# Identity products between the attention matmuls of the first slots, and the first loads issued from two engines

## The chip, the cores and the metric

One core of one Trainium2 chip runs the whole program in one launch. The metric is the device time of one execution in microseconds (us); lower is better. The core has TensorE (PE, the matrix engine), VectorE (DVE), ScalarE (ACT), GpSimd (POOL) and SyncE (SP), each with its own instruction stream, coupled by semaphores; 16 DMA engines move data between HBM and the on-chip memory. The kernel uses DMAs that SP, ACT or POOL start.

## The reference, cut to what matters

Three stages follow one another for each of 4 batches, all in fp32:

```python
# attention: 8 heads, 768 positions, head size 48
for t in range(S):
    state = alpha[:, :, t, :, None] * state + einsum('bhd,bhe->bhde', k[:, :, t], v[:, :, t])
    y[:, :, t] = einsum('bhd,bhde->bhe', q[:, :, t], state)
# token and channel mixer on x = y as (4, 768, 384)
u = x + (relu(xT @ w_tok1) @ w_tok2)T          # 768 -> 256 -> 768
x = u + relu(u @ w_ch1) @ w_ch2                # 384 -> 1536 -> 384
# channel mix with a shift by one position
k = relu(xk @ w_k); out = sigmoid(xr @ w_r) * ((k * k) @ w_v)
```

## The kernel before

**Attention in slots.** A batch's attention is cut into 6 chunks of 128 positions (c) times 4 pairs of heads (p), 24 steps in all; step i is chunk i // 4, pair i % 4. A pass over one batch has 28 slots. In each slot every engine does its share of several steps at once: in the first pass (r = 0) slot s holds the transposes of step s, the scores of step s - 2 and the output of step s - 3 (`steps_of`). Each engine's order is written out by hand in its `attention_part`. On TensorE, in slot s of the first pass:

- `attention_scores` (L519, L523): one transpose of the decayed keys and one fp32 product of 96 rows by 256 columns, after ScalarE has written `qbd`.
- `transposes` (L505): three fp32 transposes of q, k and alpha of a pair of heads, each by the identity `ident`. The first step waits for `consts_g` >= 3 (the identity is made by GpSimd), `consts_v` >= 2 and `pair_loaded` >= 48, the next one and then every fourth for `qka_loaded` of its chunk.
- `attention_out` (L543, L547, L550): four products of 48 columns, from chunk 1 on one of 96 columns with the running state, and one of 96 columns for the state.

VectorE does, per slot: the mask (L931, after the scores), the two scans of alpha (L896, L898, after the transposes), L905, L908 and L911 that scale q and k, then the state (L942 or L945) and the low part of the output (L950). ScalarE spreads q (L757, after L911), copies keys (L751) and the high part of the output (L747). GpSimd masks the state (L418) and makes the low parts of the weights (L412).

**The first pass stands alone.** In r = 0 nothing but attention runs, beside the loading and splitting of the mixer's weights, and, after slots 10, 14, 18 and 22 and at the end, three or six products of 384 columns, `early_token_up` (L588). In passes 1 to 3 each slot of attention is interleaved with a slot of the mixer of the batch before (L577, L608, L620, L636), which is much more matmul work. After pass 3 comes the mixer of the last batch, then the channel mix.

**Loads.** All loads of the first pass are issued by SP, in program order, and the waits in between are SP's own: first q, k and alpha of the first two heads of chunk 0 (L320, `pair_loaded`), then q, k, alpha of its other six heads (L300, `qka_loaded[0]`) and its v (L308), two pieces of weights (L317), then chunk 1, two more pieces, chunk 2, and mu (L328). Later chunks are loaded every fourth slot. Three buffers hold chunks 0, 1 and 2 (`chunk_buffer`). ScalarE issues no DMA. TensorE's results go to eight banks; `b_ring[1]` is a bank that nothing uses in the first pass before the mixer begins.

Of the kernel before, what the change touches and what calls it, by code (L numbers as in the profile page):

```python
# [13 lines left out]
def attention_mixer_channel_mix(nc, q, k, v, alpha, w_tok1, w_tok2, w_ch1, w_ch2,  # L14
# [7 lines left out]
    P = 128  # L22
    B, H, S, D = q.shape
# [28 lines left out]
    with ctx:  # L52
        def sb(name, shape, dt=F32):
            return ctx.enter_context(nc.sbuf_tensor(name, shape, dt))
# [29 lines left out]
        def wr_w(n, kt):  # L84
# [26 lines left out]
        ident = sb("ident", [P, P])  # L111
# [8 lines left out]
        qka3 = [[words[:, n * DM:(n + 1) * DM].rearrange("p (h d) -> p h d", h=H) for n in range(3)]  # L120
                for words in (qka[0], qka[1], free_words[0])]
        qbd = free_words[1][:, 0:4 * P].rearrange("p (n t) -> p n t", n=2)
        vt3 = [vt[0][:, :], vt[1][:, :], mixed[:, 0, :]]
# [9 lines left out]
        b_ring = [bank[3], bank[4]]  # L133
# [32 lines left out]
        consts_g = sem("consts_g")  # L166
# [3 lines left out]
        pair_loaded = sem("pair_loaded")  # L170
        qka_loaded = [sem(f"qka_loaded{n}") for n in range(3)]
        v_loaded = [sem(f"v_loaded{n}") for n in range(3)]
# [99 lines left out]
        def is_first(r):  # L272
            return isinstance(r, int) and r == 0
# [7 lines left out]
        @block.sync  # L281
        def _(sp):
            def last_use(r, c):

                if is_first(r):
                    return NP * (c - 2)
                if c >= 2:
                    return STEPS * r + NP * (c - 1)
                if isinstance(r, int) and r == 1:
                    return NP * (NC - 2 + c)  # L290
                return STEPS * (r - 1) + NP * (NC - 1 + c)

            def load_qka(b, r, c):

                buf, _ = chunk_buffer(r, c)
                if not is_first(r) or c >= 3:
                    sp.wait_ge(tr_done, last_use(r, c))
                for n, t in enumerate((q, k, alpha)):
                    h0 = 2 if is_first(r) and c == 0 else 0
                    sp.dma_start(qka3[buf][n][:, h0:H, 0:D],  # L300
                                 t[b, h0:H, c * P:(c + 1) * P, :].rearrange("h p d -> p h d"))\
                      .then_inc(qka_loaded[buf], 16)

            def load_v(b, r, c):
                buf, _ = chunk_buffer(r, c)
                if not is_first(r) or c >= 3:
                    sp.wait_ge(y_done, last_use(r, c))
                sp.dma_start(vt3[buf].rearrange("p (h d) -> p h d", h=H),  # L308
                             v[b, :, c * P:(c + 1) * P, :].rearrange("h p d -> p h d")).then_inc(v_loaded[buf], 16)

            def load_piece(n):
                dst, loaded, _ = staging(n)
                if n >= NALL - 2:
                    sp.wait_ge(tile_done, TILES * (B - 1) + KT + 2 * KC)
                elif n >= NRAW:
                    sp.wait_ge(w_lo_ready, n - NRAW + 1)
                sp.dma_start(dst.rearrange("p (k n) -> p k n", k=piece_size(n)[0]), PIECES[n][0]).then_inc(loaded, 16)  # L317

            for n, t in enumerate((q, k, alpha)):
                sp.dma_start(qka3[0][n][:, 0:2, 0:D], t[0, 0:2, 0:P, :].rearrange("h p d -> p h d"))\  # L320
                  .then_inc(pair_loaded, 16)
            for c in range(3):
                load_qka(0, 0, c)
                load_v(0, 0, c)
                for n in range(NRAW * c // 2, min(NRAW * (c + 1) // 2, NRAW)):
                    load_piece(n)
            for n, m in enumerate((mu_k, mu_r)):
                sp.dma_start(mu[:, n, :], m.rearrange("(c p) -> p c", p=P),  # L328
                             allow_slow_non_contiguous=True).then_inc(mu_loaded, 16)

            for s in range(SLOTS):

                rc, c = divmod(s // NP + 2, NC)
                if s % NP == 0 and s > 0 and (rc, c) < (1, 1):
                    load_qka(rc, rc, c)
                rc, c = divmod((s - 3) // NP + 2, NC)
                if (s - 3) % NP == 0 and s > 3 and (rc, c) < (1, 1):
                    load_v(rc, rc, c)
                for n in pieces_in(s):
                    if n + NRAW < NMIX:  # L340
                        load_piece(n + NRAW)
            load_qka(1, 1, 1)
            load_v(1, 1, 1)

            def load_chunks(r, first, last):
                for c in range(first, last):
                    load_qka(r, r, c)
                    load_v(r, r, c)

            with sp.Fori(1, B - 1) as r:  # L350
                load_chunks(r, 2, NC)
                load_chunks(r + 1, 0, 2)
            load_chunks(B - 1, 2, NC)


            for n in range(NMIX, NALL):
                load_piece(n)


            def load_x2(b, half):  # L360
                sp.wait_ge(x2_stored[half], 16 * b + 16)
                lo = half * HT - half
                sp.dma_start(x2_in[half][:, :, 1 - half:HT + 1],
                             x2_dram[b, :, lo:(half + 1) * HT].rearrange("(c p) t -> p c t", p=P))\
                  .then_inc(x2_loaded[half], 16)

            def store_out(b, half):
                for m in range(TM):
                    sp.wait_ge(y_ready, TM * (2 * b + half) + m + 4)
                    t0 = half * HT + m * P  # L370
                    sp.dma_start(out[b, t0:t0 + P, :], y_out[:, m, :]).then_inc(y_stored[m], 16)
                for m in range(TM):
                    sp.wait_ge(y_stored[m], 16 * (2 * b + half + 1))
                sp.sem_inc(y_free, 1)

            sp.wait_ge(consts_v, 6)
            for half in range(2):
                load_x2(0, half)
            with sp.Fori(0, B - 1) as b:
                for half in range(2):  # L380

                    sp.wait_ge(mixed_ready, 2 * KC * (2 * b + half + 1))
                    load_x2(b + 1, half)
                    store_out(b, half)
            for half in range(2):
                store_out(B - 1, half)
# [100 lines left out]
        @block.tensor  # L487
        def _(pe):
            PASSES = ((0, 0), (0, 1), (1, 0))

            def transposes(r, i):
                c, p = step(i)
# [16 lines left out]
            def attention_scores(r, i):  # L509
# [14 lines left out]
                else:  # L524
                    pe.wait_ge(split_ready, 3 * (STEPS * (r - 1) + i + 1))
                    for n, (a, b) in enumerate(PASSES):
                        mm = nc.tensor.matmul(scores, ks[a][0:W2, :], qs[b][0:W2, :], start=(n == 0), stop=(n == 2))  # L527
# [27 lines left out]
            def attention_part(r, s):  # L555
                tr, sc, yo = steps_of(r, s)
                if not is_first(r) and yo is not None:
                    attention_out(r, yo)
                if sc is not None:
                    attention_scores(r, sc)  # L560
                if tr is not None:
                    transposes(r, tr)
                if is_first(r) and yo is not None:
                    attention_out(r, yo)
# [6 lines left out]
            def token_up(b, m):  # L571
# [3 lines left out]
                for n in range(3 * NC):  # L575
                    i, j = PASSES[n // NC]
                    mm = nc.tensor.matmul(dst, tok1_w(i, n % NC, m), x[j][:, n % NC, :],  # L577
# [3 lines left out]
            def early_token_up(c):  # L581
# [4 lines left out]
                pe.wait_ge(xlo_ready, NP * (c + 1))  # L586
                for k, (i, j) in enumerate(PASSES):
                    mm = nc.tensor.matmul(b_ring[0][:, 0:HT], tok1_w(i, c, 0), x[j][:, c, :],  # L588
# [4 lines left out]
            def token_down(b, half, m):  # L593
# [7 lines left out]
                for n in range(3 * KT):  # L601
                    kt, (i, j) = n // 3, PASSES[n % 3]
                    if t == KT:
# [8 lines left out]
            def channel_up(b, j):  # L612
# [5 lines left out]
                for n in range(3 * KC):  # L618
                    a, c = PASSES[n // KC]
                    mm = nc.tensor.matmul(dst, ch1_w(a, n % KC, jj), u[c][:, n % KC, half * HT:(half + 1) * HT],  # L620
# [20 lines left out]
            def mixer_part(b, s):  # L641
# [7 lines left out]
                else:  # L649
# [3 lines left out]
                    if s > FIRST_UNIT:  # L653
                        channel_down(b, s - FIRST_UNIT - 1)

            for s in range(SLOTS):
                attention_part(0, s)
                if s >= 2 * NP + 2 and (s - 2) % NP == 0:
                    early_token_up((s - 2) // NP - 2)
            early_token_up(NC - 1)  # L660
# [62 lines left out]
        def _(act):  # L723
# [88 lines left out]
            def mix_next(nxt, half):  # L812

                if nxt is not None:
                    for n in range(KC + 1):
                        mix_step(nxt, half, n, 0, KC - 1)

            for s in range(SLOTS):
                attention_part(0, s)
                for n in pieces_in(s):  # L820
                    split_hi(n)
# [302 lines left out]
```

## Time and profile before

| what | us |
|---|---|
| median of 3 runs | 779.77 |
| lowest, highest | 778.67, 794.02 |
| the profiled execution, its own time | 785.57 |
| its span from the first to the last instruction | 783.9 |
| TensorE busy | 768.6 (98%) |
| VectorE, ScalarE, GpSimd busy | 469.9, 303.3, 127.7 |

The profiler recorded one execution. The page gives the busy time of each engine, the span in 40 equal slices with the granted clock of TensorE (PEclk, tenths of full speed; full is 2.4 GHz), the DMA queues, and the chain that ended last, followed back from the last instruction. Besides the page, the trace can be asked for instructions in order of time, for the chain of waits in order of time, for busy time by stretch, and for who waited for whom. Ends of matmuls are modelled since they are pipelined, so a busy TensorE is not one at its peak; the distance from start to start is the safer measure.

### The profile page before, as it was taken

What the parts mean: (1) busy time and instruction counts of PE and PEld (TensorE: products, weight loads), DVE (VectorE), ACT (ScalarE), POOL (GpSimd) and SP (SyncE); (2) the same over time, 40 slices, a digit from 0 to 9 for tenths busy, and PEclk for the clock granted to TensorE, in tenths of its full rate; (3) what the DMA queues carried; (4) which work ended last, traced back from release to release, by engine and by line L of the source; (5) the groups of instructions that cost most, each with busy time, mean ns of one, the idle gap of its engine ahead of it and who ended that gap; (6) DMA issues with size and microseconds to landing.
All of it is one profiled execution on the core that took longest, in us unless ns stands there. A gap on an engine that the chain in (4) does not pass through costs nothing.

```text
span 783.9 us, 13623 instructions
## 1 busy us (share of the span) xinstructions
PE 768.6 (98%) x4792; PEld 755.0 (96%) x4792; DVE 469.9 (60%) x1379; ACT 303.3 (39%) x843; POOL 127.7 (16%) x174
## 2 busy tenths in 40 slices
PE   6999999999999999999999999999899999999998
PEld 5988899999999999999999999999899999999998
DVE  5696877773777776387777431334663653653751
ACT  3475333332333333143333222234653643643641
POOL 1475333110013210012311043001000000000000
PEclk9999999999999999999999999999999999999999
DMA  9675222222122222122240004201010110110000
GB/s 201 142 176 127 42 41 43 71 41 41 41 56 46 42 71 42 40 43 41 41 108 18 1 31 152 73 5 61 11 50 31 41 50 30 40 50 30 5 26 30
DMA packets 114502, 43.77 MB, mean 56 GB/s; under 512 B 101776, under 2 KB 111632, under 8 KB 114448
## 3 DMA queue, kind: packets, MB, share of 16 engines
q1 hardware_dynamic: 113296, 38.36, 20.4%
q0 software_dynamic: 1152, 4.72, 1.6%
q8 instruction: 31, 0.51, 0.3%
q14 instruction: 23, 0.19, 0.1%
HBM read 33.63 MB, written 9.44 MB: 55 GB/s over the span
## 4 chain that ended last, share of the span: by engine, by line
PE 87%; DVE 8%; ACT 3%; issue 1%; DMA 0%; SPq 0%; DVEq 0%; ACTq 0%
PE bank L636 19%; PE bank L620 18%; PE bank L701 13%; PE bank L679 12%; PE bank L688 4%; PE bank L543 4%; PE bank L505 4%; PE bank L527 3%; PE bank L547 2%; PE bank L577 2%; PE bank L523 2%; PE bank L550 2%; PE bank L608 2%; ACT qs_hi L757 1%; DVE qs_lo L921 1%
## 5 line engine op out<-in xcount | busy, mean ns | idle before, releaser
L757 ACT ACTIVATE qs_hi<-qkd,rhead 96x128 fp32r<-96x128 f32 x144 | 50.1, 395 | 152.2 <-DVE qkd L911 152.2
L975 DVE SCALAR_TENSOR_TENSOR hid_lo<-bank,hid_hi 128x384 fp32r<-128x384 f32 x96 | 52.8, 550 | 68.2 <-ACT hid_hi L765 68.2
L418 POOL TENSOR_TENSOR state<-state,own 96x96 f32<-96x96 f32 x80 | 31.0, 388 | 258.7 <-DVE state L945 183.2
L765 ACT ACTIVATE hid_hi<-bank 128x384 fp32r<-128x384 f32 x96 | 46.0, 479 | 68.9 <-PE bank L620 68.9
L620 PE MATMUL bank<-u_hi,wch_hi 128*128 128x384 f32 x288 | 71.4, 356 | 0.0
L851 ACT ACTIVATE relu_k<-bank 128x384 f32<-128x384 f32 x64 | 31.5, 491 | 101.2 <-PE bank L679 83.5
L921 DVE SCALAR_TENSOR_TENSOR qs_lo<-qkd,rhead,qs_hi 96x128 fp32r<-96x128 f32 x144 | 45.9, 358 | 35.5 <-ACT qs_hi L757 35.5
L620 PE MATMUL bank<-u_lo,wch_hi 128*128 128x384 f32 x288 | 65.8, 336 | 0.0
L636 PE MATMUL bank<-hid_lo,wch_hi 128*128 128x384 f32 x288 | 65.5, 335 | 0.0
L620 PE MATMUL bank<-u_hi,wch_lo 128*128 128x384 f32 x288 | 65.5, 335 | 0.0
L636 PE MATMUL bank<-hid_hi,wch_hi 128*128 128x384 f32 x288 | 65.4, 334 | 0.0
L636 PE MATMUL bank<-hid_hi,wch_lo 128*128 128x384 f32 x288 | 65.4, 334 | 0.0
L1091 DVE TENSOR_TENSOR x_half<-bank,x_half 128x384 f32<-128x384 f32 x24 | 13.4, 557 | 76.0 <-PE bank L701 74.7
L543 PEld LDWEIGHTS bank<-vt,relu_k 128*128 128x128 f32 x352 | 54.0, 203 | 1.9 <-DVE relu_k L931 1.8
L747 ACT ACTIVATE x_hi<-bank 128x96 fp32r<-128x96 f32 x96 | 23.8, 248 | 79.5 <-PE bank L550 62.5
L1074 DVE TENSOR_TENSOR relu_k<-relu_k 128x384 f32<-128x384 f32 x64 | 35.7, 558 | 27.8 <-ACT relu_k L851 24.8
L505 PE MATMUL bank<-ident,qka 128*96 128x128 f32 x264 | 46.4, 287 | 5.8 <-DMA qka<-in_alpha 5.8
L543 PE MATMUL bank<-vt,relu_k 128*128 128x48 f32 x352 | 50.9, 270 | 0.8 <-DVE relu_k L931 0.8
L620 PEld LDWEIGHTS bank<-u_lo,wch_hi 128*128 128x128 f32 x288 | 51.7, 188 | 0.0
L620 PEld LDWEIGHTS bank<-u_hi,wch_lo 128*128 128x128 f32 x288 | 51.5, 188 | 0.0
L636 PEld LDWEIGHTS bank<-hid_hi,wch_hi 128*128 128x128 f32 x288 | 51.2, 188 | 0.1
L636 PEld LDWEIGHTS bank<-hid_hi,wch_lo 128*128 128x128 f32 x288 | 51.3, 188 | 0.0
(116 smaller groups left out, 1799.0 us busy)
## 6 DMA issues: line engine op xcount, KB each, us to landing
w_raw<-in_moe_w_ch SPq DMA_DIRECT2D x12, 384.0 KB, 3.3
x_scratch<-x_half POOLq DMA_DIRECT2D x8, 576.0 KB, 3.5
out<-x_half SPq DMA_DIRECT2D x24, 192.0 KB, 1.9
vt<-in_v SPq DMA_DIRECT2D x22, 192.0 KB, 2.7
qka<-in_q SPq DMA_DIRECT2D x21, 192.0 KB, 2.8
qka<-in_k SPq DMA_DIRECT2D x21, 192.0 KB, 3.6
qka<-in_alpha SPq DMA_DIRECT2D x21, 192.0 KB, 3.8
qka<-x_scratch SPq DMA_DIRECT2D x4, 577.5 KB, 3.9
```

What stands on the lines that cost most here:

```text
L505: mm = nc.tensor.transpose(transposed_qka(r, i)[:, n * P:(n + 1) * P], qka3[qb][n][:, 2 * p:2 * p + 2, :].rearrange("p h d -> p (h d)"), i ...
L543: mm = nc.tensor.matmul(y_ps[:, h * D:(h + 1) * D], am[:, i % 2, h * P:(h + 1) * P], vt3[vb][:, p * W2 + h * D:p * W2 + (h + 1) * D], star ...
L620: mm = nc.tensor.matmul(dst, ch1_w(a, n % KC, jj), u[c][:, n % KC, half * HT:(half + 1) * HT], start=(n == 0), stop=(n == 3 * KC - 1))
L636: mm = nc.tensor.matmul(b_acc[m][:, 0:HT], ch2_w(a, jj, m), hid[c][:, j % HJ, :], start=(jj == 0 and n == 0), stop=(jj == NJ - 1 and n == 2))
L679: mm = nc.tensor.matmul(dst, wk_w(a, n % KC, j), mix_out[0][c][:, n % KC, :], start=(n == 0), stop=(n == 3 * KC - 1))
L701: mm = nc.tensor.matmul(bank[m][:, 0:DM], k2[a][:, n % NF, m * P:(m + 1) * P], wv_w(c, n % NF), start=(n == 0), stop=(n == 3 * NF - 1))
L757: nc.scalar.activation(dst[0:W2, h * P:(h + 1) * P], qkd[0:W2, first_of(i), :], ACT.Copy, scale=rhead[0:W2, i % 4, h:h + 1])\
L765: nc.scalar.activation(dst, b_ring[t % 2][:, 0:HT], func).then_inc(tile_hi, 1)
L851: nc.scalar.activation(relu_k[:, j % 2, :], b_ring[j % 2][:, 0:HT], ACT.Relu)\
L921: nc.vector.scalar_tensor_tensor(qs[1][0:W2, cols], qkd[0:W2, first_of(i), :], rhead[0:W2, i % 4, h:h + 1], qs[0][0:W2, cols], ALU.mult, A ...
L975: ins = nc.vector.scalar_tensor_tensor(dst, src, 0.0, hi, ALU.max, ALU.subtract)
L1074: nc.vector.tensor_tensor(relu_k[:, j % 2, :], relu_k[:, j % 2, :], relu_k[:, j % 2, :], ALU.mult).then_inc(k2_ready, 1)
```

## The change

ScalarE's stream now begins with three DMA issues: k of the first two heads of chunk 0, k of its other six heads, and v of chunk 0. SP issues q and alpha of the first two heads, then q and alpha of the other six, then goes straight to the first pieces of weights and to chunk 1. TensorE waits at its start for the identity, and issues four products of the identity by itself (fp32, 128 by 128, into `b_ring[1]`, which nobody reads), two more after slot 0, and one after each of slots 1 to 5: eleven in all. No engine waits for them otherwise.

```diff
-                    h0 = 2 if is_first(r) and c == 0 else 0
-                    sp.dma_start(qka3[buf][n][:, h0:H, 0:D],
-                                 t[b, h0:H, c * P:(c + 1) * P, :].rearrange("h p d -> p h d"))\
+                    sp.dma_start(qka3[buf][n][:, :, 0:D], t[b, :, c * P:(c + 1) * P, :].rearrange("h p d -> p h d"))\
                       .then_inc(qka_loaded[buf], 16)
...
-            for n, t in enumerate((q, k, alpha)):
+            for n, t in ((0, q), (2, alpha)):
                 sp.dma_start(qka3[0][n][:, 0:2, 0:D], t[0, 0:2, 0:P, :].rearrange("h p d -> p h d"))\
                   .then_inc(pair_loaded, 16)
+            for n, t in ((0, q), (2, alpha)):
+                sp.dma_start(qka3[0][n][:, 2:H, 0:D], t[0, 2:H, 0:P, :].rearrange("h p d -> p h d"))\
+                  .then_inc(qka_loaded[0], 16)
             for c in range(3):
-                load_qka(0, 0, c)
-                load_v(0, 0, c)
+                if c > 0:
+                    load_qka(0, 0, c)
+                    load_v(0, 0, c)
...
+            WARM = (4, 2, 1, 1, 1, 1, 1)
...
+            def keep_warm(count):
+
+                for _ in range(count):
+                    nc.tensor.matmul(b_ring[1][:, 0:P], ident[:, :], ident[:, :], start=True, stop=True)
+
+            pe.wait_ge(consts_g, 3)
+            keep_warm(WARM[0])
             for s in range(SLOTS):
                 attention_part(0, s)
+                if s + 1 < len(WARM):
+                    keep_warm(WARM[s + 1])
...
+            act.dma_start(qka3[0][1][:, 0:2, 0:D], k[0, 0:2, 0:P, :].rearrange("h p d -> p h d"))\
+               .then_inc(pair_loaded, 16)
+            act.dma_start(qka3[0][1][:, 2:H, 0:D], k[0, 2:H, 0:P, :].rearrange("h p d -> p h d"))\
+               .then_inc(qka_loaded[0], 16)
+            act.dma_start(vt3[0].rearrange("p (h d) -> p h d", h=H),
+                          v[0, :, 0:P, :].rearrange("h p d -> p h d")).then_inc(v_loaded[0], 16)
             for s in range(SLOTS):
                 attention_part(0, s)
```

## Rows read from the trace of the kernel before

**Rows 1.** The page: head, busy time, granted clock in 40 slices
```profile
span 783.9 us, 13623 instructions
...
PE 768.6 (98%) x4792; PEld 755.0 (96%) x4792; DVE 469.9 (60%) x1379; ACT 303.3 (39%) x843; POOL 127.7 (16%) x174
...
PEclk9999999999999999999999999999999999999999
```

**Rows 2.** Busy time by stretch: span, us busy per engine (instructions), PEclk, DMA share, GB/s
```profile
13.70:33.00 19.30, 19.30 (x85) 17.28 (x85) 13.69 (x50) 9.26 (x28) 7.17 (x11) 1.00 0.83 186
40.00:60.00 20.00, 19.54 (x150) 17.52 (x149) 19.64 (x81) 14.04 (x46) 16.15 (x18) 1.00 0.72 178
```

**Rows 3.** Chain of waits in order of time, slots 4 to 12: start us, us, what
```profile
13.74 0.73 PE bank L505 x3
...
25.57 0.64 PE bank L505 x3
...
28.82 0.64 PE bank L505 x3
...
38.64 0.33 PE bank L505 x3
```

**Rows 4.** The same chain, slot 14 and VectorE's mask of two slots, four apart
```profile
42.01 0.34 PE bank L505 x3
...
48.88 0.36 DVE relu_k L931
...
56.88 0.36 DVE relu_k L931
```

**Rows 5.** Instructions of TensorE in order of time, products of L588: start us, us
```profile
34.44 0.52 PE L588 MATMUL bank<-x_lo,wtok_hi 128*128 128x384 f32 x1
```

**Rows 6.** All engines in order of time, slot 26 and after
```profile
59.21 0.33 PE L588 MATMUL bank<-x_lo,wtok_hi 128*128 128x384 f32 x1
...
67.23 0.52 PE L588 MATMUL bank<-x_lo,wtok_hi 128*128 128x384 f32 x1
```

**Rows 7.** Busy time by stretch, where PEclk changes
```profile
64.80:65.00 0.20, 0.20 (x3) 0.20 (x3) 0.02 (x1) 0.15 (x1) 0.20 (x1) 0.50 1.50 120
...
68.20:68.40 0.20, 0.20 (x4) 0.20 (x3) 0.00 (x0) 0.20 (x1) 0.20 (x1) 1.00 0.77 284
```

**Rows 8.** All engines in order of time, the first 14 us
```profile
0.81 1.28 ACT L757 ACT_TABLE_LOAD   x1 [0.81 <-PEq L1112]
...
1.32 0.46 SPq L320 DMA_DIRECT2D qka<-in_k  x1
1.36 0.29 POOL L394 TENSOR_SCALAR_AFFINE_SELECT ident<-ident 128x128 f32<-128x128 f32 x1 [0.23 <-POOL own L392]
...
4.02 0.92 SPq L308 DMA_DIRECT2D vt<-in_v  x1
...
4.08 0.85 PE L505 MATMUL bank<-ident,qka 128*96 128x128 f32 x3 [4.08 <-DMA qka<-in_alpha]
...
6.63 0.88 PE L505 MATMUL bank<-ident,qka 128*96 128x128 f32 x3 [1.71 <-DMA qka<-in_alpha]
...
7.42 2.69 SPq L300 DMA_DIRECT2D qka<-in_alpha  x1
...
13.60 0.45 PEld L505 LDWEIGHTS bank<-ident,qka 128*96 128x96 f32 x3 [0.58 <-DMA qka<-in_alpha]
```

**Rows 9.** Busy time by stretch of 1 us, the start of the loads
```profile
3.00:4.00 1.00, 0.00 (x0) 0.00 (x0) 0.00 (x0) 0.00 (x0) 0.00 (x0) 1.00 0.59 103
4.00:5.00 1.00, 0.85 (x3) 0.44 (x3) 0.00 (x0) 0.00 (x0) 0.00 (x0) 1.00 1.16 216
```

**Rows 10.** The chain of waits, two instructions each, in slot 8 or 9
```profile
27.92 0.91 PE bank L523 x2
...
30.18 0.51 PE bank L547 x2
```

## The prediction

> **What bounds the kernel now.** The page comes first. TensorE is busy 98% of the span and PEclk reads full speed in every slice [rows 1]. That would leave the change nothing, since it removes no matmul. But the change touches only the first few slots of the first pass, so I asked for busy time there. From 13.7 to 33 us TensorE is busy without a gap, and VectorE 13.69 us of 19.30; from 40 to 60 us, on the same kind of slots, VectorE is busy 19.64 us of 20 and TensorE is no longer full [rows 2]. The same work thus has two bounds at two times.
>
> The chain of waits in order of time gives the pace. The transposes of slot 4 start at 13.74 and those of slot 8 at 25.57, 2.96 us a slot; from slot 8 to 9 it is 3.25 us [rows 3]. Four slots of VectorE's mask later on lie 48.88 to 56.88 apart, 2.00 us a slot [rows 4]. Why TensorE needs more at first is seen on one form of instruction, a product of 384 columns: 0.52 us at 34.44, 0.33 us at 59.21 and again 0.52 us at 67.23 [rows 5, 6]. Around the last of these PEclk stands at 0.50, from 64.8 to 68.2 us [rows 7]. So 0.52 us is the duration at the low level, 1.2 GHz, and the 1.00 that PEclk shows for the first 37 us is wrong: TensorE ran at 1.2 GHz there, and PEclk only follows from the first recorded change. The transposes show it too, 0.64 us for three in slot 8 and 0.33 us in slot 12 [rows 3]. The clock rose soon after the first three 384-column products.
>
> **The loads.** Slot 0's transposes start at 4.08 us and slot 1's at 6.63, both released by the load of alpha; slot 4's at 13.60 also come after 0.58 us that end with the load of alpha of chunk 1, which SP issued at 7.42 [rows 8]. The DMA share is 0.59 from 3 to 4 us and full from 4 us on [rows 9]: up to there the issuing limits, afterwards the DMA engines do.
>
> **The change, part by part.**
> 1. *Split issue.* One issue on SP takes 0.46 us (k of the pair), that of v 0.92 us [rows 8]. Alpha of the pair is issued one place earlier: slot 0 gains about 0.5 us. Alpha of the rest is issued two places earlier; three issues leave SP, but only 0.41 us of share was free from 3 to 4 us and about all of the time before 3, so slot 1 gains between 0.4 and 1.1 us, I take 0.8. Chunk 1 follows the freed issues: at most the whole of about 2.0 us that SP gives up (two issues of k at about 0.5 and one of v at 0.92) and at least nothing, if the DMA engines are full anyway; I take 1.0 us, which is about the share that was idle before 4 us. Slot 4 goes from 13.74 to about 12.7.
> 2. *ScalarE.* Three issues of 0.46 to 0.92 us, some 1.9 us, stand ahead of its first work, beside a table load of 1.28 us that now begins at 0.81 [rows 8]. Its first activation waits for slot 0's transposes and for VectorE, well past 5 us, so I cost them at nothing. If the table load comes first, k of the pair is issued 1.28 us later and slot 0 loses what it gained, about 0.5 us; the later slots keep theirs.
> 3. *Eleven identity products.* No row shows one. It is an fp32 product that goes as two instructions, of 128 columns each. At the low clock the nearest pairs take 0.51 us for 96 columns and 0.91 us for 256 [rows 10]; I take 0.55, nearer to the first, and half of it at full clock. Four of them take 2.2 us from 1.65, where the identity is ready (1.36 + 0.29, [rows 8]), to 3.9: they hide behind the load that releases slot 0, or push it by 0.3 us. The two after slot 0 (1.1 us) fill the gap to slot 1, 1.71 us idle before [rows 8]. Those after slots 1 to 3 come before slot 4, which the load of chunk 1 releases. Only those after slots 4 and 5 are in nothing's shadow while the clock is low: 1.1 us. At full clock VectorE's 2.00 us a slot covers them. The floor is zero, the ceiling all of the last seven at 0.91, 6.4 us.
> 4. *The clock.* This is where the gain is. From slot 4 to slot 14 the kernel takes 42.01 - 13.74 = 28.27 us [rows 3, 4]. At full clock VectorE sets 2.00 us a slot, 20.0 us for ten: 8.3 us less. With the 1.0 us of the loads that is 9.3. Weights and chunks are loaded at this same pace from 40 to 60 us with a DMA share of 0.72 [rows 2], so the loads don't replace the bound for long; a stall on chunk 2 or 3 would be new, and I allow it 1 us.
>
> Will the clock rise? The rows tell what went before each rise: three 384-column products in a row ahead of slot 12, and six of them before 68.2 us. From 13.7 to 33 us it stayed low though TensorE had no gap [rows 2]. The identity products are ordinary products as those were, but shorter and fewer in a row: four and then two at the start, with only the slot's transposes between, then one in each slot, where it takes the place of a gap or lengthens the slot. That is a judgement and not a sum, and it is the weakest step. I take the clock as up for good by slot 4 or 5: one slot at the low clock loses 2.96 + 0.55 - 2.00 = 1.5 us of the 9.3. That gives 7.8 us. Against the profiled execution's own 785.57 us it is 777.8; the median of the runs is 5.8 us below that execution, and I carry the difference over: 779.8 - 7.8 = 772.0. The Trainium skill, TensorE: Matmul & The Clock Gate, section What you observe, has the clock rise early in sustained matmul activity. By that rule the change would get its 9.3 us in full, but the kernel before would not have stayed low from 13.7 to 33 us; rows 2 and 3 contradict it there, so I don't lean on it.
>
> Everything after the first pass starts earlier by the same amount, since its slots wait for each other and not for a load at a fixed time.
>
> **Rivals.**
> - *The clock rises with the opening products and stays.* The first slots then are bound by latencies and loads, slot 4 still by chunk 1, so it gives the full 9.3 us: 770.5. If the fall from 64.8 to 68.2 us [rows 7] also doesn't come, another 1.7 us (half of 3.4): 768.8. This is what the skill's rule above would give. Chance 0.25.
> - *It rises and falls back, or rises late.* At full clock the first slots have gaps for VectorE, ScalarE and the loads. The fall at 64.8 us came at the end of the pass, where the slots hold no transposes any more [rows 7]. If it is up only from about slot 8, slots 4 to 8 keep their 2.96 us and pay 1.1 us for two products: 9.3 - 3.8 - 1.1 = 4.4 us, 775.4. Chance 0.15. The Trainium skill, the same page, section Why this matters for your kernels, warns that idle gaps put the clock back; the row of 64.8 us shows a fall, but with gaps of other engines' making and not of a load's.
> - *The clock stays low until the same 384-column products, so the kernel is slower.* The place is slots 4 and 5, where TensorE is the bound [rows 2] and each product is 0.55 us in its way; the products before them also fill the slack that the earlier load opened, so slot 4 hardly gains. It decides if the clock hasn't risen by slot 6: after that no product is left. Price 1.1 us, less the 0.2 us that I leave to the loads: 779.8 + 0.9 = 780.7; at the ceiling four products at 0.91 count in full, 3.6 us and 783.4. For it speaks the 20 us at low clock with TensorE without a gap. Chance 0.2.
> - *The second queue brings nothing* (the table load goes first, or the DMA engines are full): moves any of the cases by 1 us up, and is in their ranges.
>
> **How the numbers follow.** The forecast at 772.0 has 0.4, the rivals 0.25, 0.15 and 0.2. Most of it lies between 768.5 and 776; to leave out no more than 2 in 10 the range has to reach into the low-clock case: 768 to 781. A measurement of this kernel can tell about 2% from no change, 15.6 us. No case gives that: removing the low clock altogether is worth 8.3 us plus 1.7. So within 2% has 0.95, faster 0.03 (runs of one kernel differ by 15 us at times), slower 0.02.
>
> **What would show it.** Right: pairs of L523 0.46 us instead of 0.91 apart by slot 5; slots 2.00 us apart from there, VectorE nearly full from about 13 us; PEclk with a rise in the first 15 us; slot 0's transposes near 3.6 us and slot 4's near 12.7; the end of the first pass 8 to 9 us earlier and all later stages unchanged in length. Wrong: three transposes still 0.64 us in slot 8, the slots before 6 now 3.3 to 3.5 us apart; or PEclk rising and falling again before slot 8; or slots at full clock longer than 2.1 us with waits for DMA, which would make the loads the new bound.

## The result, and the profile after

| | before | after |
|---|---|---|
| median of 20 executions, us | 785.09 | 775.85 |
| lowest, highest, us | 778.24, 798.54 | 774.14, 778.76 |
| mean, us | 786.81 | 776.08 |
| profiled execution, own time and span, us | 785.57, 783.9 | 774.48, 772.6 |

The ratio is 0.9917, 95% interval 0.989 to 0.9943. It leaves out the executions of the kernel before that lie more than 1.5% above its best (789.9 us and up, six of the 20); all of them together give 776.08 / 786.81 = 0.986. So the change is a gain of 0.8% over the better executions, with the whole interval below 1, and it takes away most of the scatter: 20.3 us from lowest to highest before, 4.6 us after.

The page of the kernel after, for [rows 1]:

```profile
span 772.6 us, 13667 instructions
...
PE 758.6 (98%) x4814; PEld 745.9 (97%) x4814; DVE 467.7 (61%) x1379; ACT 302.3 (39%) x843; POOL 127.5 (17%) x174
...
PEclk9999999999999999999999999999999999999999
```

As before, neither the busy share nor PEclk tells anything of the first 37 us. Busy time by stretch (columns as in [rows 2]), for [rows 2, 9]:

```profile
3.00:4.00 1.00, 0.79 (x4) 0.51 (x4) 0.00 (x0) 0.75 (x1) 0.00 (x0) 1.00 0.95 178
4.00:5.00 1.00, 0.99 (x5) 0.98 (x6) 0.03 (x1) 0.00 (x0) 0.00 (x0) 1.00 1.30 230
13.70:33.00 19.30, 18.98 (x145) 16.67 (x144) 18.94 (x80) 13.06 (x44) 12.79 (x16) 1.00 0.91 203
40.00:50.00 10.00, 9.68 (x75) 8.74 (x74) 9.82 (x41) 6.50 (x21) 8.15 (x9) 1.00 0.80 197
```

From 13.7 to 33 us VectorE is now busy 18.94 us of 19.30, before 13.69; the stretch looks like the one from 40 us. The DMA share from 3 to 4 us is 0.95, before 0.59. The first 14 us in order of time, for [rows 8] (line numbers of the new kernel: L508 is the old L505, L662 the identity product, L299 the load of chunk 1, here its alpha):

```profile
1.71 2.08 PE L662 MATMUL bank<-ident 128*128 128x128 f32 x8 [1.71 <-POOL ident L396]
...
2.47 1.28 ACT L769 ACT_TABLE_LOAD   x1 [2.47 <-issue]
...
4.01 0.84 PE L508 MATMUL bank<-ident,qka 128*96 128x128 f32 x3 [0.23 <-DMA qka<-in_alpha]
...
4.65 0.81 PE L662 MATMUL bank<-ident 128*128 128x128 f32 x4
...
6.50 2.39 SPq L299 DMA_DIRECT2D qka<-in_alpha  x1
...
6.99 0.54 PE L508 MATMUL bank<-ident,qka 128*96 128x128 f32 x3 [1.52 <-DMA qka<-in_alpha]
...
7.36 0.39 PE L662 MATMUL bank<-ident 128*128 128x128 f32 x2
...
12.47 0.53 PE L508 MATMUL bank<-ident,qka 128*96 128x128 f32 x3 [0.35 <-DMA qka<-in_alpha]
```

Eight L662 instructions (four products) from 1.71 last 2.08 us, 0.52 us a product; the two products after slot 0 take 0.81 us and the one after slot 1 0.39 us. The clock rose during the two products after slot 0: the transposes of slot 0 still last as long as any at the low level, the two products take less than the 1.06 us of the same two at the low level ('chunk 1 before the weights', below), and the transposes of slot 1 (0.54) last about as long as any at the full one. ScalarE's table load comes behind its DMA issues and is in nobody's way. SyncE issues alpha of chunk 1 at 6.50 us, before at 7.42. Slot 4 is at 12.47 us, released by that load. The chain in order of time, slots 4, 12 and two masks four slots apart, for [rows 3, 4]:

```profile
12.47 0.55 PE bank L508 x3
...
27.76 0.34 PE bank L508 x3
...
38.65 0.36 DVE relu_k L949
...
46.64 0.36 DVE relu_k L949
```

Slot 12's transposes start at 27.76 us, before at 38.64. VectorE's pace later is the same, 46.64 - 38.65 = 7.99 us for four slots. TensorE's transposes of slots 5, 8, 12, 14, 23 and of the first slot of the next pass:

```profile
14.23 0.49 PE L508 MATMUL bank<-ident,qka 128*96 128x128 f32 x3
...
19.67 0.49 PE L508 MATMUL bank<-ident,x_half 128*96 128x128 f32 x3
...
27.59 0.49 PE L508 MATMUL bank<-ident,qka 128*96 128x128 f32 x3
...
31.59 0.49 PE L508 MATMUL bank<-ident,qka 128*96 128x128 f32 x3
...
49.76 0.49 PE L508 MATMUL bank<-ident,x_half 128*96 128x128 f32 x3
...
56.57 0.49 PE L508 MATMUL bank<-ident,qka 128*96 128x128 f32 x3
```

The same view of the kernel before, slots 14 and 23 and the first slot of the next pass:

```profile
41.85 0.49 PE L505 MATMUL bank<-ident,qka 128*96 128x128 f32 x3
...
59.99 0.49 PE L505 MATMUL bank<-ident,x_half 128*96 128x128 f32 x3
...
67.87 0.42 PE L505 MATMUL bank<-ident,qka 128*96 128x128 f32 x1
```

The span's 11.3 us come apart by these starts. To slot 4: 13.60 and 12.47, 1.1 us. From slot 4 to 14: 41.85 - 13.60 = 28.2 us before and 31.59 - 12.47 = 19.1 us after, 9.1 us. From slot 14 to 23: 18.1 and 18.2 us, nothing. From slot 23 into the next pass: 7.9 and 6.8 us, 1.1 us; the fall of the clock of [rows 7] isn't there in this execution. Nothing came back later.

### The profile page after: what moved, and what is told of

Its sections match the earlier page's. It is cut to its first block, busy times and chain, and to the rows that moved or that the text cites. A ratio compares the mean times of both kernels' runs of the same rounds, so it can differ in the third digit from the quotient of the medians.

```text
span 772.6 us, 13667 instructions
## 1 busy us (share of the span) xinstructions
PE 758.6 (98%) x4814; PEld 745.9 (97%) x4814; DVE 467.7 (61%) x1379; ACT 302.3 (39%) x843; POOL 127.5 (17%) x174
## 4 chain that ended last, share of the span: by engine, by line
PE 85%; DVE 9%; ACT 3%; issue 1%; DMA 1%; SPq 1%; DVEq 0%; ACTq 0%
PE bank L639 19%; PE bank L623 19%; PE bank L713 13%; PE bank L691 12%; PE bank L700 4%; PE bank L546 3%; PE bank L530 3%; PE bank L508 3%; PE bank L550 2%; PE bank L580 2%; PE bank L611 1%; ACT qs_hi L769 1%; PE bank L553 1%; DVE qkd L929 1%; DVE qs_lo L939 1%
## 5 line engine op out<-in xcount | busy, mean ns | idle before, releaser
L546 PEld LDWEIGHTS bank<-vt,relu_k 128*128 128x128 f32 x352 | 50.4, 190 | 1.8 <-DVE relu_k L949 1.8
L639 PEld LDWEIGHTS bank<-hid_lo,wch_hi 128*128 128x128 f32 x288 | 51.3, 188 | 0.0
L546 PE MATMUL bank<-vt,relu_k 128*128 128x48 f32 x352 | 47.9, 258 | 0.8 <-DVE relu_k L949 0.8
```

Of the source, the lines that this page charges most:

```text
L546: mm = nc.tensor.matmul(y_ps[:, h * D:(h + 1) * D], am[:, i % 2, h * P:(h + 1) * P], vt3[vb][:, p * W2 + h * D:p * W2 + (h + 1) * D], star ...
L639: mm = nc.tensor.matmul(b_acc[m][:, 0:HT], ch2_w(a, jj, m), hid[c][:, j % HJ, :], start=(jj == 0 and n == 0), stop=(jj == NJ - 1 and n == 2))
```

## The experiments

The experiments were measured in three series, each with executions of the kernel before of its own, to which its ratios refer: their medians are 783.62 us for the first four versions, 781.9 for the next four and 786.11 for the last. A difference of two medians from different series, or from the table above, is less sure than a ratio.

**Products alone.** The loads stay on SyncE.

```diff
-            for n, t in ((0, q), (2, alpha)):
+            for n, t in enumerate((q, k, alpha)):
...
-            act.dma_start(qka3[0][1][:, 0:2, 0:D], ...)
...
```

> The eleven identity products are added, all loads stay on SyncE as in the kernel before. Theory A (the clock carries the gain): TensorE's durations halve in the first 10 us of the trace, slot 4's transposes start near 13.5 us because the load of chunk 1 still releases them, slots from 5 on lie 2.0 us apart, and the executions lie at about 775 to 780 us, 1 to 2 us above the full change's 774.1 to 778.8, in a band no wider than 5 us. Rival B (the earlier loads carry the gain, the products ride along): three transposes still take 0.64 us in slot 8 and the executions scatter from 778 to 798 us as those of the kernel before do.

Measured: median 777.54 us, 776.28 to 781.31 (12 executions), ratio 0.9951 (0.9918 to 0.9983). Transposes of slots 1 and 4 in its trace:

```profile
6.59 0.53 PE L506 MATMUL bank<-ident,qka 128*96 128x128 f32 x3 [0.83 <-DMA qka<-in_alpha]
...
13.64 0.53 PE L506 MATMUL bank<-ident,qka 128*96 128x128 f32 x3 [1.92 <-DMA qka<-in_alpha]
```

The clock was up at slot 1, and slot 4 stood at 13.64 us, as before, after 1.92 us of idle TensorE: with the clock up the load of chunk 1 is a real bound. This is theory A; the highest execution lies 1.3 us above the 780 expected, and the band is 5.0 us wide. Of the two parts of the change the products alone give a gain, with the whole interval below 1.

**Loads alone.** No identity product.

```diff
-            keep_warm(WARM[0])
...
-                if s + 1 < len(WARM):
-                    keep_warm(WARM[s + 1])
```

> The loads are issued from two engines, no identity product. Theory A: slot 0 and slot 1 start no more than 0.5 us earlier or even later, slot 4 about 1.1 us earlier, the clock stays low to the first products of 384 columns at about 33 us, and the executions scatter over 15 us or more, at best 1 us under the 778.2 us that the kernel before reached. Rival B: the executions come down to about 776 us and lie close together.

Measured: median 782.87 us, 778.44 to 797.71 (12), ratio 0.9991 (0.995 to 1.0032): no gain, the scatter unchanged. Slots 1, 4 and 11:

```profile
6.76 0.88 PE L507 MATMUL bank<-ident,qka 128*96 128x128 f32 x3 [2.37 <-DMA qka<-in_alpha]
...
13.66 0.85 PE L507 MATMUL bank<-ident,qka 128*96 128x128 f32 x3
...
35.82 0.49 PE L507 MATMUL bank<-ident,x_half 128*96 128x128 f32 x3
```

Slot 1 is later than before (6.63), slot 4 not earlier (13.60), though it no longer waits for a load: at the low clock TensorE's own work of slots 1 to 3 fills the time up to it. So the 0.58 us of [rows 8] in front of slot 4, which are idle time of the weight load, had held TensorE for hardly 0.1 us: from L523 to slot 4's transposes it took 0.97 us there and 0.91 us here. My 1.1 us for slot 4 was wrong. The two parts don't add: the loads are worth nothing without the clock, and with it 777.54 - 775.85 = 1.7 us between medians, of which 13.64 - 12.47 = 1.2 us stand in the traces.

**Opening alone and slots alone.** Of the eleven products either the first six or the last five; the loads are those of the full change.

```diff
-            WARM = (4, 2, 1, 1, 1, 1, 1)
+            WARM = (4, 2)                  # opening alone
+            WARM = (0, 0, 1, 1, 1, 1, 1)   # slots alone
```

> Only the first six products stay (four ahead of slot 0, two after it), the five after slots 1 to 5 go. If the opening alone raises the clock and attention's own work then holds it up: 774 to 778 us like the full change. If the rise depends on chance and the products in the slots are what secures it: some executions at 774 us and some above 780 us, and a trace in which the durations double again between 7 and 15 us, or stay double to about 33 us.

> The six products ahead of slot 1 go, the five after slots 1 to 5 stay. If one product in a slot is enough to raise the clock: a rise between 8 and 17 us, 775 to 779 us. If the opening is what raises it: durations stay double to about 33 us, each of the last two or three products costs about 0.5 us, and the executions scatter from 778 to 798 us, not under the kernel before.

Measured: opening alone 781.5 us, 778.41 to 794.01 (12), ratio 0.9993 (0.9947 to 1.0039); slots alone 777.34 us, 775.65 to 779.04 (12), ratio 0.9939 (0.9906 to 0.9973). Opening alone, busy time by stretch, TensorE in slot 2, and the transposes of slots 6 and 8:

```profile
6.00:8.00 2.00, 1.15 (x9) 1.04 (x9) 0.81 (x3) 0.69 (x2) 0.00 (x0) 1.00 1.09 336
8.00:10.00 2.00, 1.09 (x5) 0.60 (x4) 1.93 (x10) 0.83 (x3) 0.00 (x0) 0.72 1.36 216
10.00:20.00 10.00, 10.00 (x43) 8.66 (x43) 7.11 (x27) 4.99 (x15) 1.15 (x3) 0.50 1.11 225
22.00:24.00 2.00, 2.00 (x16) 1.86 (x15) 1.59 (x6) 0.72 (x3) 1.21 (x2) 0.86 0.45 97
```

```profile
8.85 0.40 PE L522 MATMUL bank<-ident,qkd 96*128 96x96 f32 x1 [0.59 <-DVE qkd L929]
...
19.06 0.85 PE L508 MATMUL bank<-ident,qka 128*96 128x128 f32 x3
...
23.90 0.49 PE L508 MATMUL bank<-ident,x_half 128*96 128x128 f32 x3
```

The clock was full from slot 1 (0.53 us for three transposes) to about 8.9 us, fell to 0.50 and stayed there to 22.5 us. Before the fall TensorE had worked 1.15 us of the 2.00 from 6 us on, and then nothing from 8.26 to 8.85: slot 1 waits for its load and slot 2 for VectorE. Slots alone, transposes of slots 3 and 4 and the product between them:

```profile
10.95 0.85 PE L508 MATMUL bank<-ident,qka 128*96 128x128 f32 x3
...
12.71 0.57 PE L662 MATMUL bank<-ident 128*128 128x128 f32 x2
...
13.66 0.49 PE L508 MATMUL bank<-ident,qka 128*96 128x128 f32 x3
```

It rose between 12.7 and 13.1 us, at the third product (0.57 us; 0.63 at the low level, 0.41 at the full one). What carries the gain is one product a slot in slots 1 to 5: without them the opening gives nothing, and without the opening they give a gain, with the whole interval below 1. The opening is not idle weight beside them, though: 777.34 us without it, 775.85 with it, 1.5 us between medians, of which 13.66 - 12.47 = 1.2 us stand in the traces at slot 4. With the clock up only in slot 3 TensorE's own work holds slot 4 up, and the earlier load brings nothing there. The intervals of the two ratios overlap, so this share is likely and not proven. That is the second branch of the expectation for the opening, though no execution reached its 774 us, and the first for the slots.

**Transposes in place of products.**

```diff
-                for _ in range(count):
-                    nc.tensor.matmul(b_ring[1][:, 0:P], ident[:, :], ident[:, :], start=True, stop=True)
+                for _ in range(2 * count):
+                    nc.tensor.transpose(b_ring[1][:, 0:P], ident[:, :], ident[:, :])
```

> Each of the eleven identity products is replaced by two fp32 transposes of the identity, of the same 128 columns each, so TensorE's time in them stays within some 10%. If filling TensorE's gaps is what raises the clock: as the full change, 774 to 779 us in every execution. If the kind of work matters (transposes don't count like products; the kernel before stayed low for 20 us without a gap, with four transposes a slot): the clock stays low to some later point, executions scatter to 790 us and above, and the mean lies above the kernel before's best.

Measured: median 776.33 us, 774.36 to 778.66 (10), ratio 0.9937 (0.991 to 0.9965), as the full change. Extra transposes after slots 0 and 2, then attention's own of slots 3 and 4:

```profile
4.40 1.06 PE L662 MATMUL bank<-ident 128*128 128x128 f32 x4
...
9.58 0.63 PE L662 MATMUL bank<-ident 128*128 128x128 f32 x2
...
11.08 0.63 PE L508 MATMUL bank<-ident,qka 128*96 128x128 f32 x3
...
12.90 0.49 PE L508 MATMUL bank<-ident,qka 128*96 128x128 f32 x3
```

The clock rose within slot 3's transposes. My leaning in the prediction on "ordinary products as those were" is not borne out: transposes do as well. The Trainium skill, TensorE: Matmul & The Clock Gate, section Part 4: PE-mode transpose, has it that full clock doesn't engage for transposes; these runs don't bear that out for fp32 transposes that stand between attention's products: the clock was full from slot 4 on, and all ten executions lie under 778.7 us. Whether transposes raise it as early as products do is open: slot 3 in this one trace, slots 1 to 3 in the eight traces with products.

**The kernel before, traced twice more,** unchanged.

> The kernel before, unchanged, for a second trace. If its scatter from 778.2 to 798.6 us is the chance of when the clock first rises, the slot at which three transposes go from 0.64 to 0.33 us differs from the 12th of the first trace, or is the same with the same time within 1 us, and each slot at the low level costs about 0.9 to 1.25 us. If the scatter has another cause: the same slot and another time.

> The kernel before, unchanged, for a third trace; as the second.

Measured (one execution each): 778.46 us and 781.64 us. The transposes of slots 5 and 6 in the one, of slots 5 to 7 in the other:

```profile
16.42 0.85 PE L505 MATMUL bank<-ident,qka 128*96 128x128 f32 x3
...
18.24 0.49 PE L505 MATMUL bank<-ident,qka 128*96 128x128 f32 x3
```

```profile
16.32 0.85 PE L505 MATMUL bank<-ident,qka 128*96 128x128 f32 x3
...
19.14 0.71 PE L505 MATMUL bank<-ident,qka 128*96 128x128 f32 x3
...
20.82 0.49 PE L505 MATMUL bank<-ident,qka 128*96 128x128 f32 x3
```

The kernel before rises by itself, by slot 6 in the one and in slot 6 in the other, where the trace of the prediction had it at full clock only in slot 12. No product of 384 columns had run by then, so the three ahead of slot 12 were not what it takes. Slot 5's transposes start at 16.46 us in the trace of the prediction and at 16.42 in the one of 778.46 us, slot 12's at 38.48 and 29.93, those of the next pass at 67.87 and 58.92: 8.5 us more for the seven slots, 1.2 a slot, and 8.9 into the next pass. At the end 785.57 - 778.46 = 7.1 us are left, because the execution of 778.46 us has a fall of the clock of its own between 550 and 560 us (PEclk 0.83 over those 10 us), which the first doesn't have. The other differs from the first by what comes at the end of the pass (busy time by stretch; PEclk is the third number from the right):

```profile
52.00:57.00 5.00, 4.09 (x29) 3.60 (x28) 4.19 (x17) 3.50 (x10) 4.32 (x5) 1.00 0.36 101
57.00:58.00 1.00, 1.00 (x8) 1.00 (x7) 0.44 (x1) 0.09 (x1) 0.84 (x1) 0.56 0.04 9
58.00:64.00 6.00, 6.00 (x24) 5.73 (x24) 2.39 (x9) 2.70 (x6) 4.97 (x4) 0.50 0.48 137
64.00:67.00 3.00, 3.00 (x20) 2.86 (x19) 1.19 (x4) 1.14 (x4) 0.58 (x1) 1.00 1.05 244
```

The clock lay at 0.50 from about 57 to 64 us, twice as long as the 3.4 us of [rows 7], while the execution of 778.46 us has no fall in this part. Of the 3.2 us between the two, 0.8 us stand at slot 7 (20.82 and 20.06), from the later rise, and most of the rest comes with this fall: at the second set of transposes of the next pass they are 3.2 us apart (69.36 and 66.19). No run took the fall away in the kernel before alone. Executions at 792 to 798 us weren't caught in a trace; that their clock rises later still is argued, not shown. One thing speaks for it: the mean granted clock is 0.998 in executions of 778.52 and of 792.53 us alike, so what parts these two isn't a fall that PEclk records.

**What is left of the scatter.** Two more products after each of slots 24 to 27; then one after every slot.

```diff
+                if s >= SLOTS - 4:
+                    keep_warm(2)
```

> The full change, with two more products after each of slots 24 to 27. If the executions of the full change above 775.5 us come from falls of the clock at the end of the first pass: mean clock 1.000 in most runs, 774 us, nothing at 778. If they come from falls in the slots before: the same three groups at 774.3, 775.8 and 778.2 us.

```diff
-            WARM = (4, 2, 1, 1, 1, 1, 1)
+            WARM = (4, 2) + (1,) * (SLOTS - 1)
```

> The full change, with one product after every slot of the first pass. At full clock a product takes 0.2 us of slots that VectorE bounds at 2.0 us, so it should cost nothing. If falls of the clock anywhere in the pass make the scatter: all executions within 1 us of 774.3. If the added products get in TensorE's way: 1 to 5 us longer, with slots above 2.0 us.

Measured: 775.24 us, 774.76 to 777.23 (7), ratio 0.9921 (0.9886 to 0.9957); 775.22 us, 774.69 to 776.36 (8), ratio 0.9909 (0.988 to 0.9937). With the full change 15 of 20 executions lay at 774.1 to 776.1 us with a mean granted clock of 1.000 (eight) or 0.998 (seven), and five at 778.1 to 778.8 with 0.993. With the tail products five of seven had 1.000 and none 0.993, with one in every slot six of eight and none. In the same series two versions without products at the end, 'transposes in place of products' and 'chunk 1 before the weights', have three of ten each at 0.993. So the executions at 778 us come from falls, and products up to the end of the pass stop most of them. No execution at 0.993 was traced of a version with products in the slots, so where its falls lie isn't shown. What one fall at the end of the pass costs can be read in the trace of 'transposes in place of products' (776.02 us, mean clock 0.998), where the first transposes of the next pass are at the low level:

```profile
57.76 0.84 PE L508 MATMUL bank<-ident,qka 128*96 128x128 f32 x3
```

From slot 4 to the second set of transposes of the next pass it takes 65.36 - 12.90 = 52.5 us, the full change 63.82 - 12.47 = 51.4: 1.1 us for the fall. A mean of 0.998 may also be a fall far behind the change, as the second trace of the kernel before shows. Neither version lowers the best: the lowest are about 0.6 us above the full change's, since the added products aren't free. From slot 4 into the next pass the full change takes 44.1 us, with the tail products 45.1 and with a product in every slot 44.6. The median gain over 775.85 is 0.6 us, at the edge of what these few executions tell.

**Chunk 1 before the weights.** SyncE takes v of chunk 0 back and issues chunk 1 ahead of the first weights.

```diff
-            for c in range(3):
-                if c > 0:
-                    load_qka(0, 0, c)
-                    load_v(0, 0, c)
-                for n in range(NRAW * c // 2, min(NRAW * (c + 1) // 2, NRAW)):
-                    load_piece(n)
+            load_v(0, 0, 0)
+            load_qka(0, 0, 1)
+            for n in range(2):
+                load_piece(n)
+            load_v(0, 0, 1)
+            load_qka(0, 0, 2)
+            load_v(0, 0, 2)
+            for n in range(2, NRAW):
+                load_piece(n)
...
-            act.dma_start(vt3[0].rearrange("p (h d) -> p h d", h=H),
-                          v[0, :, 0:P, :].rearrange("h p d -> p h d")).then_inc(v_loaded[0], 16)
```

> The full change, but SyncE issues v of chunk 0 and chunk 1's q, k and alpha ahead of the first two pieces of weights; ScalarE issues only the two loads of k. If the load of chunk 1 bounds slot 4 (0.35 us of idle TensorE, transposes at 12.47 us after the change) and the crowd behind it slot 1 (6.99 us): slot 1 near 6.2, slot 4 near 11.3 us, executions 1 us shorter, 773.3 at best. Rival: TensorE and VectorE need these times anyway, or the pieces now come late at slot 5: no difference within 0.5 us.

Measured: 775.47 us, 773.59 to 777.11 (10), ratio 0.9928 (0.9899 to 0.9958). Slots 1 and 4:

```profile
5.79 0.88 PE L511 MATMUL bank<-ident,qka 128*96 128x128 f32 x3
...
11.24 0.49 PE L511 MATMUL bank<-ident,qka 128*96 128x128 f32 x3
```

Slot 1 came at 5.79 us instead of 6.99, slot 4 at 11.24 instead of 12.47 and without waiting for a load. The load of alpha of chunk 0 is issued at 2.33 us in both; what moved is v, from 1.87 us to 2.92, and the weights, from 2.93 us to 6.27. So one or both of these had made it late in the full change; which of them, no run tells. The best execution is 0.6 us lower, the median 0.4.

**Both together.**

> The full change with chunk 1 loaded before the first weights and two products after each of slots 24 to 27. The two gains were 0.9 us in the profiled span (slot 4 at 11.24 us for 12.47) and the absence of executions above 777.3 us. If they add up: median 774.3, highest 776.5 us. If the earlier slots only wait later for chunk 2 or the weights: not under 775.2.

Measured: 774.59 us, 773.57 to 776.63 (6), ratio 0.9865 (0.9814 to 0.9916). This is the shortest of all medians, 1.3 us under the full change's, as expected to 0.3 us. The ratio looks better than that because the kernel before took longer in this series (786.11 us, lowest 779.82). The interval still overlaps that of the full change, so it is a likely and not a proven improvement.

## Why the prediction was right and wrong

**Right: where the time is.** The low level of TensorE's clock that PEclk doesn't show, and VectorE as the next bound at 2.00 us a slot, came out. Against the profiled execution I had 7.8 us, or 9.3 with an early rise; it is 11.1. By terms: to slot 4, 1.0 forecast and 1.1 measured; slots 4 to 14, 8.3 and 9.1, since the four slots from slot 4 take less than 2.00 us (12.47 to 19.67, 1.80 each); a slot lost to a late rise, 1.5 and 0; the fall at the end, 0 and 1.1, which I had named as a possible 1.7.

**Wrong: the step onto the median.** The prediction said: "the median of the runs is 5.8 us below that execution, and I carry the difference over". The 5.8 us were not something beside the clock, they were for the most part the clock. The execution of the kernel before at 778.46 us had risen by itself by slot 6, and in the part that the change touches it had 58.92 - 56.57 = 2.4 us left to give, not 7.8 (it lies 4.0 us above the profiled execution of the change, but 1.7 to 1.9 us of them are its fall between 550 and 560 us). By taking the whole gain off a median that already held part of it, I came to 772.0; 775.85 was measured, and the lowest execution of any version with products is 773.57. The median of the kernel before itself moved from 779.77 (3 executions) to 785.09 (20). The scatter stood in the table, 778.67 to 794.02, and I took it for noise instead of asking what differs between those executions. That the change is most of all an end to that scatter, I didn't forecast.

**Wrong: no change as the likely verdict.** I set 2% as what can be told from no change and gave "within" 0.95. The change stays within 2%, but the interval, 0.989 to 0.9943, leaves no change out. The step that failed is the reading of "runs of one kernel differ by 15 us at times" as the noise of any measurement here: the scatter belongs to the kernel before, the 20 executions after lie within 4.6 us, and the interval is 0.3% to either side, not 2%.

**Right with another mechanism: the rise.** I gave 0.4 to a rise by slot 4 or 5 and 0.25 to one by the opening products that stays. The profiled execution shows the second. But with the opening alone the clock fell back at 8.9 us, which is the rival that rises and falls back; the slots' products are what kept it up. The rival with a low clock throughout (0.2), at 780.7 us, is in no trace of the change, and none of its 20 executions is above 778.76 us.

**Right with another mechanism: slot 4.** It was to come at about 12.7 us and came at 12.47, but I gave that gain to the earlier loads alone, from the 0.58 us in front of it. The loads alone leave it at 13.66 us and the products alone at 13.64: TensorE's work at the low clock and the load of chunk 1 both ended there, and only both together move it. That the number fits is in part luck.

**Mis-sized: the small terms.** Slot 0 was to gain 0.5 us and gained 0.07 in this execution (4.08 to 4.01). In the two traces with the new loads and no product ahead of it, it came at 3.55 and 3.65 us, as forecast; with the four products, which last to 3.79 us, at 3.75 to 4.04. Slot 1 was to gain 0.8 us and lost 0.36 (6.63 to 6.99); the other traces with the full change's loads have it at 6.66 to 6.85, those with all loads on SyncE at 6.58 to 6.70. Issuing v and the weights earlier put them beside the bytes that slot 1 waits for, and the 5.79 us of 'chunk 1 before the weights' fit that. A product (its pair of instructions) costs 0.42 to 0.52 us at the low clock, not 0.55, and 0.22 to 0.25 at full clock.

## What to carry to other kernels

When a short stage with many small matmuls runs twice as slow as the same stage later, compare one instruction form at both times before believing the clock row, and trace the kernel more than once: a wide scatter of whole executions may be the clock's rise falling in different slots. Here filler in the slots where TensorE waits for others was worth more than a burst ahead of the work, and it cost little where another engine bounds the slot: 0.5 us for a product in every slot of a pass. An earlier load pays only after the engine that waits for it is no longer the bound, and issuing the rest earlier can delay the bytes that are needed first.

## What the runs showed of the hardware that was not expected

- PEclk read 1.00 up to the first recorded change while three transposes took 0.85 us; in the run with the opening alone, where a fall is recorded at 8.9 us, it read 0.50 beside the same 0.85 us. The mean granted clock of an execution leaves such a stretch out too.
- The same kernel was at 2.4 GHz by slot 6 or 7 in two traces and by slot 12 in a third, with slots 0 to 5 at the same times to within 0.2 us.
- The same six opening products had raised the clock by slot 1 in four traces (the full change, products alone, opening alone, one in every slot) and not in three others (tail products, chunk 1 before the weights, both together), where it was up by slot 2 or 3. With products in the slots this hardly moved slot 4: 12.51 us with the tail products, 12.47 in the full change.
- Fp32 transposes of the identity did about as well as fp32 products of it did, 776.33 against 775.85 us.
